# Averaged attention scores on column tiles of 32: one kernel, one core of a Trainium2 chip

## What is computed

```python
# q, k, v: (4, 8, 576, 64); factor 4
q_d, k_d, v_d = means of q, k, v over 4 neighbouring positions     # 144 positions
out_d = softmax(q_d k_d^T / 8) v_d;  out_up = repeat(out_d, 4)
scores = q k^T / 8, kept where |i - j| < 4
x = out_up + softmax(scores) v                                      # 2304 tokens x 512
g = x @ w_gate;  x = (silu(g) * (x @ w_val)) @ w_out                # hidden 1536
h = x @ w_in;    out = (max(h, 0) + alpha * min(h, 0)) @ w_out2     # hidden 2048
```

## Time and profile before

| | |
|---|---|
| runs | 974.62 us median of 3 (973.73 to 976.14) |
| the profiled execution | 975.75 us, its span 974.0 us |
| PE | 948.5 us busy, 97% of the span, granted clock 1.000 |
| DVE, ACT, POOL | 515.4, 292.3, 139.0 us busy |
| last chain | PE 91%, DVE 3%, POOL 2%, DMA 2% |
| L932, all 32 pairs | 128 matmul records, 13.9 + 2.3 us |
| L924, all 32 pairs | 1536 matmul records, 18.6 + 1.5 us |

### The profile page before, as it was taken

One profiled execution on the slowest core, in us unless ns is written; L12 is line 12 of the kernel. 1 busy time (PEld: TensorE's weight loads), 2 busy tenths in 40 slices (PEclk: granted clock), 3 DMA queues, 4 the chain that ended last, 5 costly groups with the idle time before them and its releaser, 6 DMA issues.

```text
span 974.0 us, 20421 instructions
## 1 busy us (share of the span) xinstructions
PE 948.5 (97%) x7912; PEld 886.3 (91%) x7912; DVE 515.4 (53%) x1072; ACT 292.3 (30%) x759; POOL 139.0 (14%) x158
## 2 busy tenths in 40 slices
PE   5799999999999999999999999999999999999998
PEld 3789999899998999999999999999999999999997
DVE  8477555555655656565554544445445444444433
ACT  4556333332423333333334531111111111111111
POOL 5676010010000000010104840000000000000000
PEclk9999999999999999999999999999999999999999
DMA  9465221211211322212106530020010100100000
GB/s 256 146 183 174 74 70 49 85 52 49 95 48 42 95 67 75 61 59 72 47 7 198 164 100 1 1 65 1 0 65 0 65 0 0 65 0 0 32 0 32
DMA packets 31746, 63.16 MB, mean 65 GB/s; under 512 B 2992, under 2 KB 14256, under 8 KB 31664
## 3 DMA queue, kind: packets, MB, share of 16 engines
q1 hardware_dynamic: 31664, 62.02, 20.6%
HBM read 52.57 MB, written 9.44 MB: 64 GB/s over the span
## 4 chain that ended last, share of the span: by engine, by line
PE 91%; DVE 3%; POOL 2%; DMA 2%; issue 1%; ACT 1%; SPq 0%; ACTq 0%; DVEq 0%
PE ps L1025 51%; PE ps L1062 20%; PE ps L1045 14%; PE ps L976 2%; POOL w_lo L442 2%; PE ps L924 1%; DMA w_raw<-w 1%; PE ps L932 1%; PE ps L987 1%; PE ps L962 1%; DMA qk<-qk 1%; DVE h_lo L852 0%; DVE qk_d_early L699 0%; ACT w_hi L553 0%; ACT turned_early L532 0%
## 5 line engine op out<-in xcount | busy, mean ns | idle before, releaser
L1025 PE MATMUL ps<-x_hi,w_hi 128*128 128x288 f32 x768 | 232.9, 303 | 7.8 <-POOL x_lo L479 4.4
L1025 PE MATMUL ps<-x_lo,w_hi 128*128 128x288 f32 x768 | 227.2, 296 | 0.0
L1025 PE MATMUL ps<-x_hi,w_lo 128*128 128x288 f32 x768 | 226.4, 295 | 0.0
L604 ACT CAST h_hi<-hidden 128x288 fp32r<-128x288 f32 (+1 forms) x192 | 90.8, 473 | 383.7 <-DVE hidden L889 332.0
L852 DVE TENSOR_TENSOR h_lo<-hidden,h_hi 128x288 fp32r<-128x288 f32 (+1 forms) x192 | 113.1, 589 | 95.1 <-ACT h_hi L604 91.8
L1025 PEld LDWEIGHTS ps<-x_hi,w_hi 128*128 128x128 f32 x768 | 144.4, 188 | 12.2 <-issue 8.3
L1025 PEld LDWEIGHTS ps<-x_hi,w_lo 128*128 128x128 f32 x768 | 145.0, 189 | 0.0
L1025 PEld LDWEIGHTS ps<-x_lo,w_hi 128*128 128x128 f32 x768 | 144.8, 189 | 0.0
L887 DVE TENSOR_SCALAR gated<-ps,alpha_sb 128x384 f32<-128x384 f32 x96 | 59.3, 618 | 159.4 <-PE ps L1025 159.4
L1045 PE MATMUL ps<-h_hi,w_hi 128*128 128x288 f32 x384 | 115.5, 301 | 0.2
L1062 PE MATMUL ps<-w_lo,h_hi 128*128 128x512 f32 x288 | 113.2, 393 | 0.0
(11 more groups left out here) (128 smaller groups left out, 1435.5 us busy)
## 6 DMA issues: line engine op xcount, KB each, us to landing
w_raw<-w SPq DMA_DIRECT2D x68, 256.0 KB, 2.8
qk<-qk SPq DMA_DIRECT2D x30, 436.0 KB, 3.5
vsrc_one<-vsrc SPq DMA_DIRECT2D x29, 288.0 KB
vwin<-vwin SPq DMA_DIRECT2D x30, 192.0 KB, 2.4
y_t<-y_sb SPq DMA_DIRECT2D x8, 576.0 KB, 3.4
x_raw<-y_t SPq DMA_DIRECT2D x6, 768.0 KB, 5.7
out<-y_sb SPq DMA_DIRECT2D x5, 768.0 KB, 4.0
qk_early<-qk SPq DMA_DIRECT2D x2, 436.0 KB, 6.5
```

The costliest lines, as they stand in the source:

```text
L604: nc.scalar.copy(h_hi[r][:, 0:width], hidden[r][:, 0:width]).then_inc(h_hi_ready, 1)
L1025: mm = nc.tensor.matmul(out_ps, w[:, piece, 128 * k:128 * k + 128], x_parts[low][:, k, :], start=(k == 0 and n == 0), stop=(k == KC - 1 an ...
```

## The change

The averaged scores are written as six matmuls in place of two: queries 0 to 31, 32 to 63 and 64 to 71, each for both heads, each written to PSUM partitions that begin at 0, 32 or 64. The keys, the result and its place are the same. In mode 1 PE increments a new semaphore, for which nothing waits, between the wait for the averages and the first of these matmuls.

```diff
+        scores_begun = sem("scores_begun")
...
             def down_scores(k, mode):
-                for e in range(2):
-                    rows = slice(HEAD * e, HEAD * e + HEAD)
-                    last = nc.tensor.matmul(down_ps(mode, k, e), qk_d[mode][k][rows, 0:HQ], qk_d[mode][k][rows, KD0:AVERAGED],
-                                            start=True, stop=True)
+                for first in range(0, HQ, GK):
+                    end = min(first + GK, HQ)
+                    for e in range(2):
+                        rows = slice(HEAD * e, HEAD * e + HEAD)
+                        last = nc.tensor.matmul(down_ps(mode, k, e)[first:end, :], qk_d[mode][k][rows, first:end],
+                                                qk_d[mode][k][rows, KD0:AVERAGED], start=True, stop=True)
                 return last
...
                 if mode:
                     pe.wait_ge(qk_averaged, q + 1)
+                    pe.sem_inc(scores_begun, 1)
                     down_scores(k, mode)
                     local_scores(k, half, mode).then_inc(scores_ready, 1)
```

## The result

The changed kernel is slower by half a per cent, and clear of the scatter: 980.99 us median of 11 runs (976.89 to 982.43) against 975.33 us of the kernel before in 11 runs (973.73 to 977.23), ratio 1.0052, interval 1.0042 to 1.0062. The prediction named 971.2 us, a range of 967.2 to 975.0 and 0.10 for slower.

A forecast was written before the change was run, and what follows sets the result against it. PE was taken as the bound, busy in 97% of the span; 24 rounds at 0.14 us each gave 3.4 us, taking the median from 974.62 to 971.2 us, range 967.2 to 975.0.

The forecast's parts named there:

- The holes at the change of tiling: Between L932 and L924 PE loses 0.09 to 0.10 us changing how the array is cut up; this change goes.
- Full overlap of the column groups: The averaged scores' three column groups run side by side: one load of 0.03 and two passes, 0.27 us.
- 0.15 us forecast as the limit: Sign of error: L932's second passes starting later than 0.15 us after the first would mean they share the array.
- The slower rival: Column groups take turns in L932, so L924 begins 0.33 us later a round: 982.5 us, chance 0.10.
- 0.14 us a round: Gain in each round of scores, from L924 starting 0.27 instead of 0.40 us after L932.
- what L924's end does with it: L924's last 15 loads wait for instruction delivery; counted from its first issue, the end moves 0.13 us, taken as 0.14.
- my bounds, 0.06 and 0.3: Gain a round: 0.06 us if added matmuls cost delivery 0.02 each, some 0.3 if delivery never held L924 up.
- 24 rounds: Rounds of scores taken to gain: 22 between 88 and 496 us, and two of the four before.
- I count nothing, bound 0.1 us in all.: The first four pairs run before the products, where DVE sets the pace; their gain was counted as nothing.
- the instructions come late whatever L932 does, so these I count at nothing: Two rounds where 34 of L924's 48 loads start only after a break, at 174.50 and 311.74 us; no gain.
- the holes only shrink: PE's granted clock of 1.00, its 2.4 GHz level, was expected to stay.
- The increment: PE's added semaphore increment is hidden by the sequencer's 1.5 us lead; otherwise 0.04 us off each round's gain.

The follow-up runs named there:

- otherwise equal kernels: The kernel before with 64 and with 72 idle instructions added on PE ahead of the products' loop: 985.20 and 976.67 us.
- the kernel with 64 idle instructions: The kernel before with sixteen idle 72x72 matmuls added on PE ahead of the products' loop, old scores kept: 985.20 us, ratio 1.0094.

## Why the prediction was wrong, point by point

- **The holes at the change of tiling: right.** The 0.19 us before L924's loads is gone.
- **Full overlap of the column groups: right.** First passes of L935 x6 at 103.31, second from 103.45, against 0.15 us forecast as the limit. The slower rival that I had named, column groups that take turns, didn't occur: four more matmuls made the round shorter. The result came out slower, as that rival had it, but for another reason.
- **0.14 us a round: too much, 0.104 measured** (104.40 to 105.79 before, 103.08 to 104.37 after: 1.39 and 1.29; 0.104 is the difference of the medians of 22 such rounds). The 44 passes of L925 did start 0.27 us after L935's start (103.58), as forecast, but the products came back at 0.83 and not 0.79. The step that was off is "what L924's end does with it": I took the same 15 late loads, and there are 26 now. The gain lies between my bounds, 0.06 and 0.3.
- **24 rounds: 22 are seen.** From the first product to the round behind 100 us it takes 72.2 us in both kernels (32.20 to 104.40, 30.86 to 103.08). But the kernel after did its first 6 us of products there at half clock, and over the kept traces this stretch takes 70.7 to 76.1 us, so whether two rounds of block 0 count can't be told. The sum for the scores is 2.3 to 2.7 us where I had 3.4. This alone would have been within 0.3% of no change.
- **The step that failed: of the first four pairs, "I count nothing, bound 0.1 us in all."** That holds of their own time. But they are 64 more instructions ahead of a loop's head, and this moved the head to 3 instructions before a border of the stream: +5.7 us of gaps at the two jumps, and with the lower clock behind them 8.5 us between otherwise equal kernels (985.2 and 976.67). It was settled by undoing it: 8 idle instructions.
- **"the instructions come late whatever L932 does, so these I count at nothing".** I had the rows of the two broken rounds in hand, both after the same 14 loads, and read them as noise. Their break was the border, 67 instructions behind the head, and 64 were being added.
- **The clock.** I took the granted clock of 1.00 to stay, since "the holes only shrink". The two at the jumps grew, from 1.93 to 4.89 and 4.66 us, and the clock fell to half behind them.
- **The increment: right**, within 0.2%.

Open is why the start of the products scatters by more than 1 us from kernel to kernel, why half clock comes there in some kernels, and why the gaps of the kernel with 64 idle instructions are 0.6 to 1.1 us longer than the change's own at the same place. Both parts of them are longer: the jump takes 4.29 and 3.84 us of the sequencer where it took 3.79 and 3.65, and the next lot comes 3.66 and 3.37 us after the head where it came 3.07 and 2.97 after. How much of the 8.5 us is clock was not separated by a run; from the rows it is about 11 starts of 0.24 in place of 0.13 us a jump, 1.2 us each, and more behind the second gap of the kernel with 64, where half clock lasted for 5.1 us of work.

## What to carry to other kernels

Count an edit's instructions, not only their time, when they lie ahead of or inside a loop: what they cost may be paid where the loop jumps back. In a profile look for PE waits on "issue" behind a jump and for rounds that break after the same number of instructions; the distance from the loop's head to the break tells how far the head may move. Compare variants with the head at the same place (idle instructions do it), or write the loop out on every engine that jumps; writing it out on one alone leaves the next engine's jump in its place.

## What the hardware showed that I had not expected

- A jump back on PE took 3.5 to 4.3 us of the sequencer in the ten kept traces that have it. Where the stream broke at the border, the next lot of instructions came 2.8 to 3.7 us after the first (2.9 and 3.4 in the kernel before, 3.1 and 3.0 in the kernel after), whether 3, 35 or 67 instructions were left to run.
- Every gap of 4.7 to 6.0 us at a jump was followed by a stretch at about half clock. Of those from 2.0 to 2.7 us some were (2.12, 2.16, 2.67) and some weren't (2.03, 2.15, 2.30).
- Six fp32 streams of 144 elements on six tiles of two row halves and three column groups started within 0.04 us of each other, and four passes of the local scores started before their second passes.
